# An attention and MLP chain on one core: the last blocks of the second batch are turned by DMA and VectorE instead of TensorE

## The reference, cut to what matters

```python
h = np.maximum(xt @ w_tok1, 0.0) @ w_tok2            # mix over tokens
u = x + h.transpose(0, 2, 1)
x = u + np.maximum(u @ w_ch1, 0.0) @ w_ch2           # 512 -> 1536 -> 512
u = x + np.real(fft(fft(x, axis=1), axis=2))
un = (u - mu) / np.sqrt(var + 1e-06)                 # per token, over channels
out = u + np.maximum(un @ w_ch1, 0.0) @ w_ch2        # 512 -> 2048 -> 512
```

## Time and profile before

| | |
|---|---|
| median of 3 runs | 564.48 us (564.41 to 566.05) |
| the profiled execution: its own time | 564.52 us |
| its span | 562.6 us |
| busy: TensorE matmuls, VectorE, ScalarE, GpSimd | 556.3, 367.6, 252.3, 256.9 us |
| granted TensorE clock, mean of the core | 0.999 |

### The profile page before, as it was taken

How to read it: one execution, slowest core, us unless ns; L and a number is a source line. 1 busy time by engine, 2 the same in 40 slices (tenths; PEclk the granted TensorE clock), 3 DMA queues, 4 the chain that set the end, 5 groups by cost and what they waited for, 6 DMA issues and landing times.

```text
span 562.6 us, 9227 instructions
## 1 busy us (share of the span) xinstructions
PE 556.3 (99%) x3388; PEld 496.3 (88%) x3388; DVE 367.6 (65%) x641; ACT 252.3 (45%) x507; POOL 256.9 (46%) x285
## 2 busy tenths in 40 slices
PE   8999999999999999999999999999999999999998
PEld 6889889979998999898888899988988989998996
DVE  6975867575777885467989854679863634344324
ACT  2665335545545444335555443355454433434430
POOL 3663435334667654223777542236663333233311
PEclk9999999999999999999999999999999999999999
DMA  8970303822222212012022120120222221221142
GB/s 322 409 283 2 113 0 112 212 90 54 70 76 76 75 57 74 21 57 75 19 72 76 60 76 20 56 76 19 76 76 75 76 74 58 75 76 57 38 150 112
DMA packets 31950, 50.55 MB, mean 90 GB/s; under 512 B 2714, under 2 KB 12962, under 8 KB 31906
## 3 DMA queue, kind: packets, MB, share of 16 engines
q1 hardware_dynamic: 31312, 48.12, 26.3%
q0 software_dynamic: 448, 1.71, 1.0%
q10 hardware_dynamic: 146, 0.13, 0.1%
HBM read 45.24 MB, written 3.15 MB: 86 GB/s over the span
## 4 chain that ended last, share of the span: by engine, by line
PE 92%; DMA 2%; DVE 2%; SPq 1%; ACT 1%; issue 1%; ACTq 0%
PE banks L1283 15%; PE banks L1284 15%; PE banks L1282 15%; PE banks L1562 12%; PE banks L1564 12%; PE banks L1565 12%; PE banks L1355 2%; PE banks L1306 2%; PE banks L1343 2%; DMA qTs<-qT_dram 1%; PE banks L1399 1%; PE banks L1331 1%; PE banks L1419 1%; DMA th<-u 1%; PE banks L1380 1%
## 5 line engine op out<-in xcount | busy, mean ns | idle before, releaser
L414 POOL TENSOR_TENSOR w2l<-raw,w2h 128x512 fp32r<-128x512 f32 x56 | 74.0, 1323 | 141.1 <-ACT w2h L552 141.1
L1562 PE MATMUL banks<-th,al 128*128 128x384 f32 x392 | 131.9, 336 | 1.7 <-DVE snap L1156 1.4
L1564 PE MATMUL banks<-tl,ah 128*128 128x384 f32 x392 | 132.3, 337 | 0.0
L1565 PE MATMUL banks<-th,ah 128*128 128x384 f32 x392 | 132.0, 337 | 0.0
L552 ACT ACTIVATE snap<-banks 128x384 f32<-128x384 f32 x84 | 41.1, 489 | 124.8 <-PE banks L1565 124.8
L827 DVE TENSOR_TENSOR al<-raw,ah 128x512 fp32r<-128x512 f32 (+1 forms) x112 | 88.3, 808 | 5.1 <-ACT ah L552 3.9
L1156 DVE TENSOR_TENSOR snap<-banks,snap 128x384 f32<-128x384 f32 x84 | 46.3, 552 | 56.3 <-PE banks L1565 56.2
L1562 PEld LDWEIGHTS banks<-th,al 128*128 128x128 f32 x392 | 73.6, 188 | 9.7 <-DVE snap L1156 2.2
L1564 PEld LDWEIGHTS banks<-tl,ah 128*128 128x128 f32 x392 | 73.5, 188 | 6.1
L1565 PEld LDWEIGHTS banks<-th,ah 128*128 128x128 f32 x392 | 73.6, 188 | 0.0
L414 POOL TENSOR_TENSOR raw<-raw 128x256 f32<-128x256 f32 x84 | 69.3, 841 | 2.2
(11 more groups left out here) (187 smaller groups left out, 908.3 us busy)
## 6 DMA issues: line engine op xcount, KB each, us to landing
raw<-w1b_dram SPq DMA_DIRECT2D x16, 512.0 KB, 3.3
raw<-w2b_dram SPq DMA_DIRECT2D x32, 256.0 KB, 2.9
raw<-w2a_dram SPq DMA_DIRECT2D x24, 256.0 KB, 2.9
kTs<-kT_dram SPq DMA_DIRECT2D x8, 384.0 KB, 8.8
qTs<-qT_dram SPq DMA_DIRECT2D x8, 384.0 KB, 9.2
vns<-vn_dram SPq DMA_DIRECT2D x8, 384.0 KB, 8.9
kns<-kn_dram SPq DMA_DIRECT2D x8, 384.0 KB, 9.8
raw<-w1a_dram SPq DMA_DIRECT2D x6, 512.0 KB, 3.5
```

What stands on the lines that cost most here:

```text
L414: return nc.gpsimd.tensor_tensor(o, i0, i1, ALU.subtract)
L1562: mm(o[:, 0:HALF], al[:, a, cols], th[b][:, t, k, :], start=start and k == 0, stop=False, skip_group_check=True)
L1564: mm(o[:, 0:HALF], ah[:, a, cols], tl[b][:, t, k, :], start=False, stop=False, skip_group_check=True)
L1565: last = mm(o[:, 0:HALF], ah[:, a, cols], th[b][:, t, k, :], start=False, stop=(k == 1), skip_group_check=True)
```

## The change

`MOVED` becomes (1, 3): the blocks of ch 3 are made without TensorE too. `ln_norm` of batch 1 writes the normed rows into `normed`, which lies over the block tiles of batch 1; `move_normed(n, quadrants)` copies them with 16 DMAs of 32 partitions x 2 x 128 elements per n (48 in all) into `moved`; `turn_squares(3, n)` turns them. The blocks of n = 0 are made at j = 6 and those of n = 1 and 2 at j = 7, in the closing order that ch 1 has at j = 5; before they were at j = 4, 5, 6. The up-weights of ch 3 are loaded by four DMAs each. For ch 1, `moved` gets another layout, quadrants 2 and 3 are copied at p = 2 behind its first and second down-weights, and the three turns come at the ends of p = 2, 3 and 4.

```diff
-        {**FOURIER, 5: BLOCKS[1], 6: BLOCKS[2]}, {}]
+        {2: FOURIER[2], 3: FOURIER[3], 6: BLOCKS[0],
+         7: (None, None, ("b1", 1), ("b2", 1), ("b1", 2), ("b2", 2))}, {}]
-MOVED = 1
+MOVED = (1, 3)
...
+            alias = ExitStack()
+            nb.append(sb(alias, f"normed{b}", [L, 4, 2, HALF]))
+            alias.close()
...
-                if ch == MOVED:
+                if ch in MOVED:
                     for i in range(L // Q):
                         rows = w1[2 * j:2 * j + 2, :, i * L:(i + 1) * L].rearrange("m p n -> (m p) n")
...
+            def move_normed(n, quadrants):
+
+                t = TILES[MOVED[1]][n]
+                sp.wait_ge(un_ready, NC + 2 * n + 2)
+                for i in quadrants:
+                    to = slice(i * Q, (i + 1) * Q)
+                    for j in range(L // Q):
+                        rows = slice(j * Q, (j + 1) * Q)
+                        sp.dma_start(moved[to, j, t:t + NA + 1:NA, :, :].rearrange("p n k c -> p n (k c)"),
+                                     normed[n][rows, :, i, :]).then_inc(s_norm_moved[n], 16)
+
             for p in range(1, NP):
+                late = p - FIRST[2]
...
+                if late == 6:
+                    move_normed(0, (3,))
+                if late == 7:
+                    move_normed(2, (0, 1))
+                sp.wait_ge(w2l_ready, 2 * p - 1)
+                down_weights(p, 0)
+                if p in (1, 2):
+                    move_squares(p)
+                if late == 5:
+                    move_normed(0, (0,))
+                if late == 6:
+                    move_normed(1, (0, 1))
+                if late == 7:
+                    move_normed(2, (2,))
+                sp.wait_ge(w2l_ready, 2 * p)
+                down_weights(p, 1)
                 if p == 2:
                     move_squares(3)
...
+                if late == 5:
+                    move_normed(0, (1, 2))
+                if late == 6:
+                    move_normed(1, (2, 3))
+                if late == 7:
+                    move_normed(2, (3,))
...
-                closing = ch == 1 and j == 5
+                closing = (ch, j) in ((1, 5), (2, 7))
...
-                if ch + 1 == MOVED and j == 2:
-                    turn_squares(1)
+                if ch == 2 and j == 7:
+                    turn_squares(3, 2)
                 side_lo(ch, j, 1)
...
-                if ch + 1 == MOVED and j in (1, 2):
-                    turn_squares(0 if j == 1 else 2)
+                if ch == 0 and 2 <= j <= 4:
+                    turn_squares(1, j - 2)
+                if ch == 2 and j in (5, 6):
+                    turn_squares(3, j - 5)
...
-                if units[i] is None or ch + 1 == MOVED:
+                if units[i] is None:
                     return
                 what, n = units[i]
+                if what in ("b1", "b2") and ch + 1 in MOVED:
+                    return
```

More of the change, by code:

```diff
@@ L99, in w1_loaded @@
         def w1_loaded(p):
-            return 16 * sum(L // Q if place(q)[0] == MOVED else 1 for q in range(p + 1))
+            return 16 * sum(L // Q if place(q)[0] in MOVED else 1 for q in range(p + 1))
         NI = 4
@@ L188, in build @@
             tl[b] = sb(ctx, f"tl{b}", [L, 7, 2, HALF], f32r)
-        moved = f(th[MOVED % B][:, T2:T4 + 1, :, :]).rearrange("p s k n -> p (s k n)").rearrange(
-            "p (n j k c) -> p n j k c", n=NC, j=L // Q, k=KD)
+        moved = f(th[MOVED[0] % B][:, T2:T4 + 1, :, :]).rearrange("p s k n -> p (s k n)").rearrange(
+            "p (j n k c) -> p j n k c", n=NC, j=L // Q, k=KD)
+        normed = [nb[MOVED[1] % B][:, :, :, t * L:(t + 1) * L].rearrange(
+            "p (i s) k n -> p i (s k) n", i=2) for t in TILES[MOVED[1]]]
         warm_ready, warm_done = sem("warm_up_zeros_ready"), sem("warm_up_done")
@@ L203, in build @@
         s_moved = sem("residual_squares_moved")
+        s_norm_moved = [sem(f"normed_squares_moved_{n}") for n in range(NA)]
         b1_turned, b2_turned = sem("first_blocks_turned"), sem("second_blocks_turned")
@@ L266, in transposed, with turning @@
         def transposed(target, n, half):
-            return 2 * event(target - (1 if target > MOVED else 0), n) + half + 1
+            return 2 * event(target // 2, n) + half + 1
+        def turning(target, n):
+            return event(MOVED.index(target), n)
         def u_count(b, t):
@@ L941, in token_out, with turn_squares @@
                 nc.vector.tensor_tensor(u[:, n, :], bank[token_bank(b, t)][:, :], u[:, n, :], ALU.add).then_inc(u_ready, 1)
-            def turn_squares(n):
-                b, t = MOVED % B, TILES[MOVED][n]
+            def turn_squares(target, n):
+                b, t = target % B, TILES[target][n]
                 cols = slice(t * L, (t + 1) * L)
-                dve.wait_ge(s_moved, 16 * (L // Q) ** 2)
+                dve.wait_ge(s_moved if target == MOVED[0] else s_norm_moved[n], 16 * (L // Q) ** 2)
                 def turned(o, i, half):
-                    squares = moved[:, t + NA * i, :, 2 * half:2 * half + 2, :].rearrange("p j k c -> p k j c")
+                    squares = moved[:, :, t + NA * i, 2 * half:2 * half + 2, :].rearrange("p j k c -> p k j c")
                     return nc.vector.transpose(o.rearrange("p k (j r) -> p k j r", r=Q), squares)
@@ L1124, in ln_norm @@
                 dve.wait_ge(rstd_ready, NA * b + n + 1)
-                if n == 2:
-                    dve.wait_ge(tr_done, transposed(2 + b, 0, 1))
+                if n == 2 and b == 0:
+                    dve.wait_ge(tr_done, transposed(2, 0, 1))
                 for i in range(2):
-                    nc.vector.tensor_scalar(un[2 * (n % 2) + i], u[:, NC * b + NA * i + t, :], mv[:, b, t, i, 0:1],
+                    nc.vector.tensor_scalar(normed[n][:, i, :, :] if b else un[2 * (n % 2) + i], rows_of(b, NC * b + NA * i + t), mv[:, b, t, i, 0:1],
                                             rstd[:, b, t, i:i + 1], ALU.subtract, ALU.mult).then_inc(un_ready, 1)
@@ L1248, in _ @@
                 if closing:
-                    up_corner_lo(p + 1)
+                    if j == 5:
+                        up_corner_lo(p + 1)
                     hidden_lo(p, 4, h0l[:, second], snap[:, 1, :], h0h[:, second])
@@ L1547, in bank_read @@
                 ch, j = place(p - 1)
-                units = EMPTY if ch + 1 == MOVED else SIDE[ch].get(j, EMPTY)
+                units = SIDE[ch].get(j, EMPTY)
                 for i in (4, 2) if k == 6 else (5, 3):
-                    if units[i]:
+                    if units[i] and not (units[i][0] in ("b1", "b2") and ch + 1 in MOVED):
                         side_read(ch, units[i])
```

33 lines of the change are left out of this document (14 added, 19 removed).

## The result

The changed kernel takes **569.87 us** (median of 4 runs, 569.45 to 571.37), the kernel before, in runs beside it, 565.26 us. The ratio of the comparison is 1.0096, 95% interval 1.0075 to 1.0118: slower by about 5.4 us by the ratio, by 4.6 us between the two medians. The profiled execution of after took 569.45 us with a span of 567.6 us, against 562.6 before.

A forecast was written before the change was run, and what follows sets the result against it. TensorE was taken as the bound, busy 556.3 of 562.6 us. From the profiled 564.52 us, -2.75 - 1.7 + 5.4 + 0.4 = +1.35 gave 565.9 us, range 562.2 to 568.4.

The forecast's parts named there:

- Transposes gone, -2.75: Pairs 16 to 18: without the transposes of ch 3, 2.75 us leave TensorE.
- Wait in pair 2 gone, -1.7: Pair 2: TensorE's wait in front of S4, put down to the second `hidden_sum`, goes, saving 1.7 us.
- Up-weights in four DMAs, 0: Loading ch 3's up-weights by four DMAs costs 0; the longer issue is hidden by SP's idle time.
- n = 0 and n = 1, 0: Normed rows of n = 0 and n = 1: 0, up to 0.5 us; moves land some 3.5 us into pair 18.
- Step 1, the last moves: Pair 19: SP issues the last four moves from 6.72 us, 0.37 apart; they land at 10.4 us.
- the SP rival: SP's issue is the bound: forty small DMAs at 0.61 us or more, deciding from about 0.5; 568.0 us, chance 0.19.
- Step 2, turn and S4: Pair 19: VectorE's turn waits to 10.4 us, `hidden_sum` starts at 11.74, S4 waits 1.8 us.
- Steps 3 and 4, the blocks and the alternation: After `hidden_sum`, VectorE's blocks take 8.95 us; alternating with GpSimd adds about 2.15, so B21 and B22 are ready 11.1 later.
- a: Start of the `hidden_sum` that S4 of pair 19 waits for, forecast 11.74 us after that pair's first product.
- A12 late by +5.4: Pair 20: A12, due 17.4 us after pair 19's first product, starts at 22.8, 5.4 us late.
- Behind it, +0.4: Pairs 20 and 21, behind A12: 0.3 us from GpSimd's lateness and VectorE's residual additions, and a little for pair 21.
- its own case: The forecast's main case: 565.9 us, from 565.0 to 567.2 on its own, chance 0.40.

The follow-up runs named there:

- e1: The kernel before with only the front part of the change (residual squares' moves and turns in ch 1): ratio 0.9982 to before.
- e3: The changed kernel with the normed moves issued earlier in SP's list, none behind the last down-weights of p = 19: ratio 1.0031 to before.
- e11: e3's blocks, but the rows of n = 0 and n = 1 moved together, 32 moves in place of 48: ratio 1.0040 to before.
- e4: The changed kernel with TensorE running down products d7 to d10 ahead of S4 in pair 19: ratio 1.0115 to before.
- e5: e3, with GpSimd's sums of ch 3's n = 1 and n = 2 begun only after VectorE has made all B tiles: ratio 1.0072 to before.
- e8: The changed kernel with one n's blocks in each of pairs 17, 18, 19, moves from stage 16, turns where VectorE idles: 560.27 us, ratio 0.9931 to before.
- e12: The changed kernel with VectorE's turn of n = 2 in pair 19 put behind the blocks of n = 1: ratio 1.0045 to before.
- e6: The changed kernel with blocks of n = 0 and 1 in pair 18, n = 2 alone in pair 19, moves issued earlier: ratio 1.0033 to before.
- e7: The changed kernel with GpSimd's sums of n = 1 and n = 2 put behind VectorE's B tiles, moves unchanged: ratio 1.0115 to before.

## Why the prediction was wrong, step by step

- *Transposes gone, -2.75.* Right: -2.80.
- *Wait in pair 2 gone, -1.7.* Right in the profiled execution, -1.68; over many runs it is 1.0 (e1). A wait that ends with a DMA landing was read from a single execution and taken for its mean.
- *Up-weights in four DMAs, 0; n = 0 and n = 1, 0.* Right as such. The turn of n = 0 waited 3.42 us, to t = 3.56 of pair 18 (forecast 3.5), and delayed nothing. But the four DMAs hold SP for 2.06 us in the middle of the moves, which belongs to step 1.
- *Step 1, the last moves.* **This is the step that failed**: "With 64 pieces per DMA I am nearer to the first and take 0.37 from start to start." Measured 0.64; an issue of such a move costs nearly the same with 64 pieces of 512 B, 64 of 1 KB and 192 of 512 B. From 391.44 on SP then has 36 moves, 4 down-weights at 0.64 each (an issue of theirs takes 0.58 behind others and 0.33 alone) and 2.06 for the up-weights: 40 x 0.64 + 2.06 = 27.7 us, to 419.1. The last move started at 419.5 and ended at 420.1 (one issue took 1.37, as one takes 1.2 to 1.8 in seven of the other runs, and there was a pause of 0.3). The premise "SP issues the second down-weights of p = 19 when GpSimd is done" fell with it: GpSimd was ready at t = 6.7, SP came at t = 9.3. Landed: 14.0 for 10.4.

Nor had the earlier trace rows "few pieces": its DMA loads 128 rows of 2 KB from DRAM, twice as many as a move has, and the trace of before also has a load from DRAM of 256 pieces of 512 B on 32 partitions, at 0.45 us (first row below, durations on SP in ns). So the number of pieces doesn't order the durations. The moves have SBUF as their source and the loads DRAM; whether that is the reason no run isolates, and a load right behind moves takes 0.58 too.

```profile
L306 SPq DMA_DIRECT2D raw<-w1a_dram x24: 327/451/457, 154.6 to 244.4; - x24
```

```profile
100.82 2.56 SPq L334 DMA_DIRECT2D th<-u  x4
```

- *The bound for that step*, the SP rival (568.0, chance 0.19), named the right mechanism but priced it low: it let the last moves start near 10.1, and the last one started at 12.2. At 0.61 per entry the list above gives 10.0, so the rival's sum was sound for its number. But 0.61 is the duration of a move in the earlier trace rows; from start to start the same moves lie 0.65 apart (second row above: four in 2.56 us, the last of them 0.61). At 0.64 the list gives 11.1, and the single long issue and the pause make up the rest. With 11.1 the rival's own sum comes to 568.9, above the range. Its threshold of 0.5 was low as well: by the same list SP comes to the second down-weights later than GpSimd from 0.59 per entry on.
- *Step 2, turn and S4.* Mechanism right. S4 waits by what the landing is late: 5.3 us for 1.8.
- *Steps 3 and 4, the blocks and the alternation.* Right: a + 11.1 forecast; a + 11.0 measured in after, e3 and e11 and a + 10.9 in e4; a + 8.95 without GpSimd (e5). The Trainium skill's rule ("SBUF — State Buffer", Who interferes with whom), that the loser of the shared port blocks for a whole instruction, agrees with e3 beside e5: one `tl` of VectorE takes 1.37 us in e3 while GpSimd runs and 0.42 in e5 while it rests.
- *A12 late by +5.4.* As a function of the landing it was right: e3, whose moves land at 10.06, has 5.05, and its ratio of 1.0031 is near the forecast's (565.9 / 564.48 = 1.0025). In after it is a = 15.38, + 11.0 - 17.4 = 9.0, and 9.04 was measured.
- *Behind it, +0.4.* Between e11 (5.33 late, pairs 19 + 20 +5.38) and e3 (5.05 and +5.71) it is 0.05 to 0.7, in after 0.04. What makes the difference is whether TensorE is at the lower level when it comes out of its last wait. The forecast had no term for the clock. In after it needed none, in e4 and e5 it did.

With the measured 14.0 in place of 10.4 the forecast's own sum is 565.9 + 3.6 = 569.5; the profiled execution took 569.45. That the two meet within 0.1 us is partly luck: 0.4 was forecast behind A12 and 0.04 measured, and pair 0, which the change doesn't touch, began 0.37 later. The forecast gave its own case 0.40 and slower 0.36; the error is one duration, taken between two rows that lay a factor of 1.8 apart, by a rule (few pieces, short issue) that no row had shown and that the rows of before speak against.

Open: what in the issue of a move costs 0.59 us, where the same engine issues a load of 256 KB from DRAM in 0.33 when it stands alone. e8's first move, after 5 us of pause, took 0.59 too, so it isn't the queue behind it. Moving them from another engine's queue was not tried. Nor is it shown why the granted clock fell in e3 behind a wait of 2.13 us and not in e11 behind one of the same 2.13.

## What to carry to other kernels

Sum an issuing engine's whole list, from its last real pause, at the distance from start to start of the nearest rows of the same kind (here SBUF to SBUF), before reading any single landing; the range must hold the case in which the list never pauses. Work that depends on a landing belongs behind everything on its in-order engine that doesn't (e12), and this goes for each engine on the way: VectorE's late turn held up ScalarE's snapshots in e6, the moves held up up-weights in e11. When a wait is filled and the time doesn't move (e4), look for the later wait that the same chain sets; and two engines that hold each other off share one sum, so the cure is to put less of it into the last pair (e8), not to reorder it (e5).

## What the runs showed of the hardware

- A move of 32 partitions within SBUF takes SP 0.60 to 0.61 us of issue, 0.64 to 0.65 from start to start, with 96, 64 or 32 KB (192 or 64 pieces); landing 1.8 to 3.3 us for the normed rows. A load from DRAM of 256 KB in 128 rows takes 0.33 alone and 0.58 behind others, one of 256 pieces on 32 partitions 0.45.
- TensorE after a wait of 5.3 us: granted clock 0.71 from 420 to 425 and 0.61 from 425 to 430, products of 384 columns 0.32 us apart in place of 0.17, over by 428.8. Behind 3.93 us in e6, 3.32 in e12, 2.84 in e5 and 2.17 in e4 the first products were slow at once; behind 2.13 us in e3 they became slow only 0.9 us later, from 427.3 to 430.4, and in e11 behind 2.13 us and in e7 behind 2.02 not at all. A lower clock inside a wait for another engine cost nothing in after; behind the last wait it cost 0.7 us (e3), 1.2 (e4) and 2.8 (e5) in the profiled executions.
- An operation of VectorE on two SBUF operands beside GpSimd took 1.37 to 1.41 us where it takes 0.42 alone, and a row of three took 2.3 where it takes 1.2.
